# Attention's queries grouped by the MLP's token tiles, and the MLP started at beat 16 instead of 28, in a fused kernel

## The reference

```python
# attention: batch 4, 8 heads, 576 queries and keys, head size 64
scores = scale * q @ k.T
thresh = max(scores) - tau
scores = where(scores >= thresh, scores, -1e9) - max(scores)
attn = exp(scores); attn = attn / (sum(attn) + 1e-9)
x = (attn @ v), heads side by side          # 2304 tokens x 512
# MLP 1: 512 -> 2048 -> 512
r = maximum(x @ w_in, 0); x = (s * r * r + b) @ w_out
# MLP 2: 512 -> 2048 -> 512
h = x @ w_in2; out = (h * sigmoid(1.702 * h)) @ w_out2
```

## Time and profile before

| | |
|---|---|
| median of three runs | 1107.87 us (1107.8 to 1108.33) |
| the profiled execution | 1111.1 us, span 1109.3 us, mean granted clock 0.984 |
| TensorE busy | 1043.1 us, 94% (weight loads 920.0 us, 83%) |
| VectorE busy | 608.1 us, 55% |
| ScalarE busy | 673.2 us, 61% |
| GpSimd busy | 779.7 us, 70% |
| chain that ended last | TensorE 74%, VectorE 16%, SyncE's queue 3% |

### The profile page before, as it was taken

The page is one execution under the profiler, slowest core; times in us unless marked ns, Lnnn a source line. Parts: engine busy times, 40 slices in busy tenths (PEclk is TensorE's granted clock), DMA queues, the critical chain, the costliest instruction groups (busy, mean ns, idle before and its releaser), DMA issues.

```text
span 1109.3 us, 18120 instructions
## 1 busy us (share of the span) xinstructions
PE 1043.1 (94%) x5904; PEld 920.0 (83%) x5904; DVE 608.1 (55%) x1544; ACT 673.2 (61%) x1255; POOL 779.7 (70%) x773
## 2 busy tenths in 40 slices
PE   4878589999999899999999999999999999999998
PEld 3666478888888788887989989889999998999997
DVE  5899989998999899893222232322222223222222
ACT  4677466777677667765676666645545445454543
POOL 4666588888788778874666756667667667676673
PEclk9899799999999999999999999999999999999999
DMA  4122577777678776676333333333534444344431
GB/s 137 44 89 77 135 183 196 211 207 213 171 201 215 181 196 183 174 189 170 122 115 123 125 120 126 121 121 111 170 124 153 132 138 138 126 155 128 151 126 66
DMA packets 126621, 162.63 MB, mean 147 GB/s; under 512 B 27328, under 2 KB 68928, under 8 KB 126528
## 3 DMA queue, kind: packets, MB, share of 16 engines
q1 hardware_dynamic: 126528, 161.47, 49.6%
HBM read 124.85 MB, written 4.72 MB: 117 GB/s over the span
## 4 chain that ended last, share of the span: by engine, by line
PE 74%; DVE 16%; issue 3%; SPq 3%; POOL 1%; DMA 1%; ACT 1%; DVEq 0%; ACTq 0%; POOLq 0%
PE y_ps L449 31%; PE scores L431 25%; PE shared L431 6%; DVE scores L504 6%; PE scores L343 5%; PE scores L396 5%; DVE prob L528 4%; DVE blocks L543 3%; SPq L273 2%; PE shared L396 1%; DMA raw_out<-slabs_a 1%; DVE limit L511 1%; DVE gate L557 1%; PE shared L458 1%; POOL k_lo L788 1%
## 5 line engine op out<-in xcount | busy, mean ns | idle before, releaser
L808 POOL TENSOR_TENSOR win_lo<-raw_in,win_hi 128x512 fp32r<-128x512 f32 x192 | 288.6, 1503 | 96.6 <-ACT win_hi L669 96.5
L815 POOL TENSOR_TENSOR wout_lo<-raw_out,wout_hi 128x512 fp32r<-128x512 f32 x192 | 253.3, 1319 | 101.8 <-ACT wout_hi L676 101.8
L557 DVE TENSOR_TENSOR gate<-scores,gate 128x384 f32<-128x384 f32 x134 | 74.7, 558 | 409.0 <-ACT gate L686 298.2
L449 PE MATMUL y_ps<-wout_lo,g_hi 128*128 128x512 f32 x576 | 227.9, 396 | 0.0
L449 PE MATMUL y_ps<-wout_hi,g_hi 128*128 128x512 f32 x576 | 227.7, 395 | 0.0
L449 PE MATMUL y_ps<-wout_hi,g_lo 128*128 128x512 f32 x576 | 227.7, 395 | 0.0
L704 ACT CAST g_hi<-gate 128x384 fp32r<-128x384 f32 x192 | 98.6, 514 | 139.3 <-PE y_ps L449 138.4
L431 PE MATMUL scores<-act_hi,win_lo 128*128 128x384 f32 x536 | 180.9, 337 | 0.0
L431 PE MATMUL scores<-act_hi,win_hi 128*128 128x384 f32 x536 | 180.5, 337 | 0.0
L431 PE MATMUL scores<-act_lo,win_hi 128*128 128x384 f32 x536 | 180.0, 336 | 0.0
L637 ACT ACTIVATE prob<-scores,neg_max 128x576 f32<-128x576 f32 (+2 forms) x160 | 118.5, 741 | 92.4 <-DVE scores L504 81.8
(11 more groups left out here) (66 smaller groups left out, 1645.8 us busy)
## 6 DMA issues: line engine op xcount, KB each, us to landing
raw_in<-slabs_a SPq DMA_DIRECT2D x96, 256.0 KB, 3.0
raw_out<-slabs_a SPq DMA_DIRECT2D x96, 256.0 KB, 2.9
raw_in<-slabs_b SPq DMA_DIRECT2D x96, 256.0 KB, 2.6
raw_out<-slabs_b SPq DMA_DIRECT2D x96, 256.0 KB, 2.6
qk_raw<-qk SPq DMA_DIRECT2D x32, 576.0 KB, 4.1
prob_t<-blocks SPq DMA_DIRECT2D x144, 100.0 KB, 2.9
prob_t<-blocks SPq DMA_DIRECT2D x144, 80.0 KB, 2.6
v_sb<-v SPq DMA_DIRECT2D x16, 320.0 KB, 3.2
```

Of the source, the lines that this page charges most:

```text
L449: mm = nc.tensor.matmul(y_ps[g][:], gp[:, n % 2, toks], wp[n % RING_OUT][:], start=(f == 0 and k == 0), stop=(f == SLABS - 1 and k == 2))
L808: nc.gpsimd.tensor_tensor(win_lo[n % RING_IN][:], raw_in[:, n % 2, :], win_hi[n % RING_IN][:].bitcast(F32), ALU.subtract).then_inc(win_lo_ ...
L815: nc.gpsimd.tensor_tensor(wout_lo[n % RING_OUT][:], raw_out[:, n % 2, :], wout_hi[n % RING_OUT][:].bitcast(F32), ALU.subtract).then_inc(wo ...
```

## The change

The tiles' order now follows the MLP's tokens. A *group* is 384 queries of both heads of a pair (long: three tiles of 128 rows per head, 3 beats) or 192 (short: two tiles of 96 rows per head, 2 beats). First come the long groups of batch 0's four pairs (MLP tile 0), then the short groups of batches 0 and 1 (tile 1), batch 1's long groups (tile 2), and then batches 2 and 3 pair by pair, long and short, the last two pairs with both long groups first. There are still 160 tiles and 80 beats; MLP step 0 stands in beat 16 instead of 28, `BEATS` is 84 and `FIRST_PURE` 68.

Only the four first groups (24 tiles) are turned by TensorE instead of 40 tiles. The blocks of both heads of a group lie side by side, so that one move takes both: 16 DMAs for a long group, 12 for a short one, in runs of 192 or 128 values instead of 160; the context's streaming operand then gathers one head's runs. `prob_t` has two halves of 384 columns, and a move into a half waits for the last piece that reads it (`pieces_on`). Probability buffers are six instead of four, value buffers two instead of one; values are loaded 26 times instead of 16.

Queries and keys are loaded apart: 48 loads of 384 query columns in a ring of three, 32 loads of 576 key columns. Keys of batches 0 and 1 are kept, split, for their second use, in 8 places that lie where the second half of `act_hi` and `act_lo` comes later, and in a ring of four. A raw key lies in the place of its low part. The first head's low key part is made by VectorE instead of GpSimd.

Raw weight slabs lie in the place of their low parts, so that the rings are 4 and 5 deep; a slab load waits for matmuls of earlier steps instead of GpSimd's split. The input slab is loaded three steps ahead instead of two; the output slab is loaded one step ahead as before, but split one step later on ScalarE and GpSimd. In mixed beats ScalarE copies a finished tile's rows after the gate instead of before.

```diff
+PROBS = 6
+LONG, SHORT = 384, 192
+PIECE = SHORT
+TILES_PER_HEAD = {LONG: 3, SHORT: 2}
+ROWS = {LONG: 128, SHORT: 96}
+Q_COLS = LONG
+Q_RING = 3
...
+def groups_in_order():
+    order = [(0, p, 0, LONG) for p in range(4)] + [(0, p, LONG, SHORT) for p in range(4)]
+    order += [(1, p, 0, SHORT) for p in range(4)] + [(1, p, SHORT, LONG) for p in range(4)]
+    order += [(2, p, q0, n) for p in range(4) for q0, n in ((0, LONG), (LONG, SHORT))]
+    order += [(3, p, q0, n) for p in range(2) for q0, n in ((0, LONG), (LONG, SHORT))]
+    return order + [(3, p, q0, n) for q0, n in ((0, LONG), (LONG, SHORT)) for p in (2, 3)]
...
+def half_of(w):
+    return 0 if is_long(w - 1) else 1 - half_of(w - 1)
+def moved_into(w, a):
+    return a // 2 if is_long(w) else half_of(w)
...
+Q_LOADS = [(w, side) for w in range(len(GROUPS_OF)) for side in (range(2) if is_long(w) else range(1))]
...
+def q_split_beat(i):
+    return FIRST_BEAT[Q_LOADS[i][0]] - 2
...
+STORE, KEY_RING = 8, 4
...
+def key_slot(e):
+    batch, h = divmod(e, HEADS_PER_BATCH)
+    if batch == 0 or (batch == 1 and h >= KEY_RING):
+        return h - KEY_RING * batch
+    return STORE + h % KEY_RING
...
+def key_split_beat(e):
+    if e // HEADS_PER_BATCH == 1:
+        return PE_TILES // 2 + 1 + (e - HEADS_PER_BATCH) * 3 // 2
+    return FIRST_BEAT[TILE_AT[key_tiles(e)[0]][0]] - 3 + 2 * (e % 2)
...
-RING_IN, RING_OUT = 3, 5
+IN_HI, IN_LO, OUT_HI, OUT_LO = 3, 4, 4, 5
+IN_EARLY, OUT_EARLY = 3, 1
...
-MLP_FROM = 28
...
+MLP_FROM = 16
+def pieces_in_order():
+    pieces = []
+    for w in range(len(GROUPS_OF)):
+        after = 5 if w < PE_GROUPS or not is_long(w) else 6
+        pieces += [(w, n, FIRST_BEAT[w] + after + n) for n in range(2 if is_long(w) else 1)]
+    return pieces
...
+def pieces_on(w, half):
+    return 1 + max(piece for piece, (n, place, _) in enumerate(PIECES)
+                   if n < w and (n < PE_GROUPS or (place if is_long(n) else half_of(n)) == half))
...
-            def move_quad(h, a):
-                side = h % 2
...
+            def load_k(e):
+                if key_before(e) is not None:
+                    sp.wait_ge(scores_ready, key_tiles(key_before(e))[-1] + 1)
+                if e >= 2:
+                    sp.wait_ge(k_hi_ready, e - 1)
+                sp.dma_start(k_raw[key_slot(e)][:], k[e]).then_inc(k_loaded[e % 2], 16)
...
+            def move_quad(w, a):
+                n = 2 * TILES_PER_HEAD[GROUPS_OF[w][3]]
+                half = moved_into(w, a)
+                start = n * BLK * a if is_long(w) else LONG * half + n * BLK * a
                 if a == 0:
-                    sp.wait_ge(turned, TPH * (h + 1) - PE_TILES)
-                sp.wait_ge(context_ready, THIRDS * (h // 2 - 1) + min(a + 1, THIRDS))
-                n = QUAD_RUNS[a]
+                    sp.wait_ge(turned, FIRST_TILE[w + 1] - PE_TILES)
+                sp.wait_ge(context_ready, pieces_on(w, half))
                 for r in range(4):
                     c = len(range(r, BLOCKS, 4))
-                    sp.dma_start(prob_t[side][BLK * r:BLK * r + BLK, 0:c, RUN * a:RUN * a + n],
-                                 blocks[side][BLK * a:BLK * a + BLK, r::4, 0:n // BLK, :]
-                                 .rearrange("p c t j -> p c (t j)")).then_inc(moved[side][a], 16)
+                    sp.dma_start(prob_t[BLK * r:BLK * r + BLK, 0:c, start:start + n * BLK],
+                                 blocks[BLK * a:BLK * a + BLK, w % 2, r::4, 0:n, :]
+                                 .rearrange("p c t j -> p c (t j)")).then_inc(moved[half][a], 16)
+            def move_quads(w, beat):
+                for a in range(quads_of(w)):
+                    if beat == FIRST_BEAT[w] + (4 if is_long(w) else 3) + a // 2:
+                        move_quad(w, a)
...
+                if n >= IN_LO:
+                    sp.wait_ge(h_ready, n - IN_LO + 1)
...
+                if n >= OUT_LO:
+                    sp.wait_ge(y_step_done, n - OUT_LO + 1)
...
             def slabs(s):
-                if 2 <= s + 1 < STEPS:
+                if OUT_EARLY <= s + 1 < STEPS:
                     load_out(s + 1)
-                if 2 <= s + 2 < STEPS:
-                    load_in(s + 2)
-            load_head(0)
+                if IN_EARLY <= s + 3 < STEPS:
+                    load_in(s + 3)
+            load_k(0)
+            load_q(0)
             sp.dma_start(consts[:, 0:3], consts_in).then_inc(consts_loaded, 16)
-            load_head(1)
+            load_k(1)
+            load_q(1)
+            sp.dma_start(ident[:], ident_in).then_inc(ident_loaded, 16)
+            load_q(2)
             load_values(0)
-            sp.dma_start(ident[:], ident_in).then_inc(ident_loaded, 16)
-            for n in range(2):
-                load_in(n)
-                load_out(n)
+            load_values(1)
...
+                        if rides(piece):
+                            start = LONG * (n if is_long(w) else half_of(w))
+                            rows = prob_t[:, c, start:start + LONG].rearrange("p (a s q) -> p a s q", a=len(quads),
+                                                                              s=2)[:, :, side, :]
+                            place = place.rearrange("p (a q) -> p a q", a=len(quads))
...
+            dve.wait_ge(k_hi_ready, 1)
+            nc.vector.tensor_tensor(k_lo[key_slot(0)][:], k_raw[key_slot(0)][:], k_hi[key_slot(0)][:].bitcast(F32),
+                                    ALU.subtract).then_inc(k_lo_ready, 1)
...
             def rows_and_gate(s):
                 n = s - OUT_LAG
-                if n >= 0 and n % SLABS == SLABS - 1:
+                ended = n >= 0 and n % SLABS == SLABS - 1
+                if ended and s >= FIRST_PURE:
                     copy_rows(n)
                 if 0 <= s < STEPS:
                     gate_of(s)
+                if ended and s < FIRST_PURE:
+                    copy_rows(n)
                 if 0 <= s + 2 < STEPS:
                     slab_in_hi(s + 2)
+            split_k(0)
             act_eng.wait_ge(lower_set, 2)
             split_q(0)
-            split_k(0)
+            split_k(1)
+            split_q(1)
...
-                if 0 <= s + 1 < STEPS:
-                    slab_out_hi(s + 1)
-                for h in range(1, HEADS):
-                    if q_split_beat(h) == beat:
-                        split_q(h)
-                    if q_split_beat(h) + 1 == beat:
-                        split_k(h)
+                if 0 <= s < STEPS:
+                    slab_out_hi(s)
...
-                if 0 <= s < STEPS:
-                    slab_out_lo(s)
...
+                if 0 <= s - 1 < STEPS:
+                    slab_out_lo(s - 1)
```

More of the change, by code:

```diff
@@ new lines, with is_long @@
+GROUPS_OF = groups_in_order()
+PE_GROUPS = PAIRS_PER_BATCH
+FIRST_TILE = [2 * sum(TILES_PER_HEAD[n] for _, _, _, n in GROUPS_OF[:w]) for w in range(len(GROUPS_OF) + 1)]
+FIRST_BEAT = [tile // 2 for tile in FIRST_TILE]
+TILES = FIRST_TILE[-1]
+PE_TILES = FIRST_TILE[PE_GROUPS]
+PE_HEADS = 2 * PE_GROUPS
+TILE_AT = [(w, side, t) for w, (_, _, _, n) in enumerate(GROUPS_OF)
+           for side in range(2) for t in range(TILES_PER_HEAD[n])]
+def is_long(w):
+    return GROUPS_OF[w][3] == LONG
+def rows_of(j):
+    return ROWS[GROUPS_OF[TILE_AT[j][0]][3]]
@@ L97, in pieces_before, with piece_place, value_loads @@
     return sum(due < beat for _, _, due in PIECES)
-def act_cols(piece):
-    pair, q0, _ = PIECES[piece]
-    at = (pair // PAIRS_PER_BATCH) * SEQ + q0
-    return pair % PAIRS_PER_BATCH, slice(at, at + THIRD)
+def piece_place(piece):
+    w, n, _ = PIECES[piece]
+    batch, pair, q0, _ = GROUPS_OF[w]
+    return pair, batch * SEQ + q0 + PIECE * n
 def pieces_for(tile):
-    return 1 + max(n for n in range(len(PIECES)) if act_cols(n)[1].start < (tile + 1) * TOK)
+    return 1 + max(piece for piece in range(len(PIECES)) if piece_place(piece)[1] // TOK == tile
+                   or (piece_place(piece)[1] + PIECE - 1) // TOK == tile)
+def pieces_on(w, half):
+    return 1 + max(piece for piece, (n, place, _) in enumerate(PIECES)
+                   if n < w and (n < PE_GROUPS or (place if is_long(n) else half_of(n)) == half))
+def value_loads():
+    loads = []
+    for piece, (w, _, _) in enumerate(PIECES):
+        key = GROUPS_OF[w][0], GROUPS_OF[w][1]
+        if not loads or loads[-1][0] != key:
+            loads.append([key, piece, piece])
+        loads[-1][2] = piece
+    return loads
+VALUES = value_loads()
+VALUE_OF = {piece: i for i, (_, first, last) in enumerate(VALUES) for piece in range(first, last + 1)}
 def tiles_of(beat, lag=0):
     return range(2 * beat - lag, 2 * beat - lag + 2)
-def q_split_beat(h):
-    return max(0, (TPH * (h - 1) - 1) // 2)
 def tile_of(s):
@@ L152, in build @@
         g_lo = sbuf(ctx, "g_lo", [P, 2, TOK], F32R)
[L153 to L158 removed]
+        win_hi = [sbuf(ctx, f"win_hi{n}", [P, D_MODEL], F32R) for n in range(IN_HI)]
@@ L204, in build @@
         turned = sem("turned")
```

(4 more changed lines are left out.)

423 lines of the change are left out of this document (226 added, 197 removed).

## The result

The change made the kernel slower. Its median is 1134.03 us (four runs, 1130.35 to 1136.8) against 1108.1 us (four runs, 1107.8 to 1111.84): ratio 1.0224, 95% interval 1.0185 to 1.0263. The forecast was 1085 us, with a range of 1076 to 1100. The profiled execution took 1136.8 us, its span 1135.0.

What follows compares the result with a forecast made beforehand. TensorE was busy nearly throughout; VectorE set attention-alone beats and mixed beats without a context piece, TensorE those with one. Terms -54.4 + 27.9 - 1.0 + 1.5 + 3 + 1 - 1 = -23.0 us from 1107.87 gave 1085, range 1076 to 1100.

Steps and rivals of the forecast that it cites:

- main claim: MLP from beat 16: twelve beats leave the attention-alone stage, saving 54.4 us; twelve more mixed beats cost 27.9 us.
- Step (6): Moves in SyncE's queue: first riding context at beat 17 stalls 3 us; short groups' later cycles cost 1 us in all.
- SyncE rival: Moves waiting for context pieces, slab loads behind them: 1.0 us slip in each of 28 moved groups gives 1113; chance 0.05.
- Steps (1) and (4): First stage: 16 alone beats take 75.0 us against 129.4; moving 16 tiles' turns from TensorE to VectorE costs nothing more.
- Step (5): GpSimd's split operations, beats 13 to 23: smaller query splits at 1.0 us; delay between 0 and 4, taken as 1.5 us.
- second rival: GpSimd becomes late in the mixed stage: 27 beats without a piece end 0.5 us late, 13 us lost, 1098; chance 0.15.
- Step (3): Start: first k difference goes to VectorE, gain taken as 1.0 us; by the shared-port rule it would be 0.
- both criteria: Forecast is wrong if quiet five-beat stretches reach 34.5 us or more, or the first stage keeps over 80 us.
- step (7): Output slabs split a beat after their load is issued, deeper rings: net between -5 and +3 us, taken as -1.

Runs made afterwards that it cites:

- four small edits: Changed kernel with GpSimd's normalisation on 128 partitions, tail copied ahead of the exponent, query and value loads one beat later, most short riding pieces one beat later: 1084.66 us.
- the run with later loads: Changed kernel with only SyncE's query loads one beat later and value loads one beat after the context that frees the buffer: 1124.86 us.

## Why the prediction was wrong

**The main claim held.** Attention beats cost less beside MLP steps than alone. The forecast gave this trade 54.4 - 27.9 = 26.5 us; starting at beat 16 instead of 28 gained 33 among the stalls and 41 without them. These two are gains over the regrouped kernel, whose alone beats are dearer, so the 26.5 wasn't measured as it stands. With four small edits the kernel runs in 1084.66 us where 1085 was forecast; its profile has 71.2, 107.3, 360.5 and 530.3 us for the four stretches, against 75.0, 109.4, 361.6 and 530.6. That isn't a hit: the forecast was for the kernel as written.

**Step (6), the moves, failed, and it is the largest miss.** It named the right places, beat 17 and the short groups' later cycles, and then charged 3 + 1 us. Letting the short pieces ride a beat later gave 25. Four of its inputs were too kind. Landing was taken as the median of 3.0 us; on the chain it was 4.40 at beat 29, 5.07 at beat 17, and 4.95 in the run with later loads. For the first wait its own sum gave 4 to 5, and I took 3 by an argument about TensorE's slack; it was 9.54:

```profile
108.04 3.42 PE L555 MATMUL scores<-prob_t,v_sb 128*64 128x192 f32 x20 [9.54 <-DMA prob_t<-blocks]
```

The sum also left out a key, a value and a query load, which SyncE issues between the first eight moves and the slab loads (98.25 to 99.80 us), and it had TensorE at this context 6.5 to 7.6 us after the last alone piece, where it came after 5.6 (92.9 to 98.5). And a wait was priced at its own length. Behind each, the context also ran 3.4 to 3.5 us instead of 1.85, 1.6 more, at a granted clock of 0.50 to 0.53.

**The loads' waits were left out of step (6).** The SyncE rival's count had only moves and slab loads (18.2 + 4.3 of 32.9 us), and found over 8 us to spare per cycle. But the spare time isn't where the moves need it: a query load waited up to 8.3 us for GpSimd, a value load up to 5.3 for a context, with moves behind both. Moving the loads gave 9 us. This is the rival "SyncE's queue falls behind", which had 0.05: its place was right, its slips came fewer and larger than its 1.0 us in each of 28 groups, and it deserved far more, since I had found zero slack myself. The slab loads' own waits, for hidden units (L433, 40.7 us) and outputs (L441, 28.1), also stand ahead of moves; they weren't tried apart.

**Steps (1) and (4), "it costs nothing".** The alone beats were carried over from a kernel with five tiles to a head. With three, the bank of the tails is needed again one turn after its last write. This cost 12 us; with the copy ahead of the exponent the stage took 72.0 us, within the forecast's 75.0. The operation was the same and the rows true; what changed was how soon its buffer is wanted, which a mean per beat doesn't show.

**Step (5) and the second rival failed in their place.** They charged GpSimd, and GpSimd wasn't late: in the five-beat stretch it has 28.75 us, as before. VectorE was, 33.34 of 35.9 against 30.87 of 32.9, through g_lo. The Trainium skill (SBUF — State Buffer, "SBUF: two separate sides") says that the two hold the port pair in turn for a whole operation. The rows agree, 0.55 becoming 1.75 while wout_lo takes its 1.29. I had read the rule as a cost to GpSimd because the earlier trace rows shows VectorE winning. The losing case, 1.77 us at 156.27, was in the trace of before and I didn't look for it. Worth about 10 us; the step priced GpSimd's delay at 0 to 4, the rival at 13, and neither had VectorE losing the port.

**What held.** Step (3): the first exponent stands at 9.6 us instead of 10.7, 1.1 earlier, where 1.0 was forecast (in runs with the same start it stood at 9.6 to 10.4). The reason was partly another one: the two first differences still run one after the other, because VectorE is at its memsets until then, but both are shorter, as the timeline shows:

```profile
4.98 0.99 POOL L950 TENSOR_TENSOR q_hl<-q_raw,q_hl 128x384 fp32r<-128x384 f32 x1 [4.15 <-ACT q_hl L784]
...
6.28 0.76 DVE L654 TENSOR_TENSOR k_lo<-k_raw,k_hi 128x576 fp32r<-128x576 f32 x1
```

They took 1.40 us each before. So the term wasn't 0, although the two did run one after the other. The row also confirms the 1.0 us that step (5) took for a query split: 0.99. The last 530 us are unchanged. The quiet beat of 5.9 us is still there (5.92 at beats 22, 26 and 28), and both criteria flagged rightly: five beats took 35.9 us (34.5 was the limit), the first stage 85.4 (80). The three turning sets take 38.0, 37.5 and 38.0 us per five beats (34 to 38, 50 to 54, 66 to 70), inside the 37 to 39 named. The size of step (7) wasn't taken apart.

**The range.** Its top, 1100, came from adding each step's own upper bound. Three causes, the tails' copy, the loads' waits and VectorE's loss of the port, had no term and so no bound. Three of the four causes sit where an order written by hand has a wait with no spare beat.

## What to carry to other kernels

When a change regroups work, list every buffer and ring and count how long each new owner has between its last writer and its next use; mean beat times from the old grouping don't contain that. In an in-order queue, spare time in the sum says nothing: walk the queue with its waits, take the slow landings and not the median, and where a step comes out at zero slack, give it a beat more or charge it the whole wait and the matmuls at the lower clock behind it. Look on both engines of a shared port for who loses, and in the old trace for the rare long instance of a short operation.

## What the runs showed that was not expected

Who gets the port between a key split and wout_lo goes with an earlier operation of GpSimd's queue: behind normalisations of 128 partitions VectorE's g_lo takes 0.54 to 0.58 us, behind ones of 96 or 112 it takes 1.73 to 1.77 against the same operations, and a wait of GpSimd for its own result turns that back to 0.55 to 0.57. It was worth about 10 us here. In the kernel before, every key split in that place stood behind normalisations of 128, and only one g_lo of 57 came behind 96 partitions and a query split, so there was next to nothing to gain.

Waits cost twice. In the changed kernel, after a wait of 2.4 to 9.5 us TensorE's next 20 context matmuls take 3.1 to 3.5 us instead of 1.85, at a granted clock of 0.50 to 0.57 instead of 1.00. It isn't so for every such wait: in the run with the later loads one of 3.22 us had 1.85 behind it.
